# One fused attention and expert kernel: the experts' first block put through its first layer inside the attention's last batch, and the k and q stacks loaded one after the other

## What is computed

```python
for t in range(S):
    ar, ai = (a_re_n[:, :, t, :, None], a_im_n[:, :, t, :, None])
    new_re = ar * S_re - ai * S_im
    new_im = ar * S_im + ai * S_re
    kv = np.einsum('bhd,bhe->bhde', k[:, :, t], v[:, :, t])
    S_re, S_im = (new_re + kv, new_im)
    y[:, :, t] = np.einsum('bhd,bhde->bhe', q[:, :, t], S_re)
```

```python
logits = x @ w_gate + modality_bias[modality_id]
e_idx = np.argmax(logits, axis=1)
for e in range(E):
    mask = e_idx == e
    h = np.maximum(x[mask] @ w1[e], 0.0)
    out[mask] = gate_w[mask, None] * (h @ w2[e])
```

## Time and profile before

| what | value |
|---|---|
| median of three executions | 1009.62 us (1009.51 to 1011.83) |
| the profiled execution | 1016.24 us |
| its span, first to last instruction | 1014.5 us |
| PE busy | 826.1 us (81%) |
| DVE, ACT, POOL busy | 501.3, 345.9, 128.8 us |
| mean granted TensorE clock | 0.939 of full |

### The profile page before, as it was taken

The page is one execution under the profiler, slowest core; times in us unless marked ns, Lnnn a source line. Parts: engine busy times, 40 slices in busy tenths (PEclk is TensorE's granted clock), DMA queues, the critical chain, the costliest instruction groups (busy, mean ns, idle before and its releaser), DMA issues.

```text
span 1014.5 us, 11936 instructions
## 1 busy us (share of the span) xinstructions
PE 826.1 (81%) x4633; PEld 679.2 (67%) x4633; DVE 501.3 (49%) x920; ACT 345.9 (34%) x676; POOL 128.8 (13%) x126
## 2 busy tenths in 40 slices
PE   0059500399899997969999999989999999999996
PEld 0034200168788786838888888877898989898986
DVE  2599999959696853565345444544111111111110
ACT  6921101153535332425244524533222222222220
POOL 0201100000000302220000000000323232323232
PEclk9999855599897998989999999999999999999998
DMA  9934300475646456225244134214100000000000
GB/s 381 372 121 156 109 0 0 96 194 157 172 125 171 114 128 213 87 83 162 86 156 154 35 123 156 68 60 143 46 32 1 32 1 32 1 32 1 32 0 32
DMA packets 48054, 102.99 MB, mean 102 GB/s; under 512 B 12145, under 2 KB 30450, under 8 KB 45682
## 3 DMA queue, kind: packets, MB, share of 16 engines
q1 hardware_dynamic: 41810, 81.97, 26.3%
q0 software_dynamic: 5632, 18.94, 5.2%
q10 hardware_dynamic: 544, 1.20, 0.5%
HBM read 64.12 MB, written 18.95 MB: 82 GB/s over the span
## 4 chain that ended last, share of the span: by engine, by line
PE 69%; DVE 18%; ACT 5%; issue 3%; DMA 2%; another core or an unknown queue 1%; ACTq 1%; POOL 1%; SPq 0%; POOLq 0%; DVEq 0%
PE moe_bank L1573 18%; PE moe_bank L1574 18%; PE moe_bank L1575 18%; PE bank L989 4%; PE bank L1017 3%; DVE rows L783 3%; DVE rows L784 2%; PE bank L1034 2%; DVE gates L786 2%; PE bank L947 2%; PE bank L1038 1%; DVE gates L787 1%; DVE gates L773 1%; PE bank L997 1%; DMA gates<-a_im 1%
## 5 line engine op out<-in xcount | busy, mean ns | idle before, releaser
L1565 DVE TENSOR_TENSOR u_sb<-x_in,moe_bank 128x512 f32<-128x512 f32 x48 | 33.0, 688 | 229.9 <-PE moe_bank L1575 229.9
L1573 PE MATMUL moe_bank<-xT_hi,w_hi 128*128 128x512 f32 x312 | 124.1, 398 | 1.3 <-DVE xT_lo L1499 1.3
L1575 PE MATMUL moe_bank<-xT_hi,w_lo 128*128 128x512 f32 x312 | 123.8, 397 | 0.0
L1574 PE MATMUL moe_bank<-xT_lo,w_hi 128*128 128x512 f32 x312 | 123.5, 396 | 0.0
L1400 POOL TENSOR_TENSOR hid_lo<-u_sb,hid_hi 128x512 fp32r<-128x512 f32 x48 | 62.2, 1296 | 404.0 <-ACT hid_hi L1461 404.0
L960 PE MATMUL bank<-early_w_out,early_w3T 128*128 128x384 f32 x128 | 44.9, 507 | 64.7 <-DMA early_w_out<-w_out 61.3
L960 PEld LDWEIGHTS bank<-early_w_out,early_w3T 128*128 128x128 f32 x128 | 24.7, 197 | 84.4 <-issue 62.8
L952 PE MATMUL bank<-consts 128*128 128x512 f32 x36 | 18.4, 667 | 76.8 <-DVE gates L849 76.8
L1476 ACT COPY x_in<-moe_bank 128x512 f32<-128x512 f32 x48 | 28.3, 589 | 150.3 <-PE moe_bank L1575 150.3
L1439 ACT ACTIVATE hid_hi<-moe_bank 128x512 fp32r<-128x512 f32 x56 | 33.5, 597 | 129.2 <-PE moe_bank L1575 129.2
L1573 PE MATMUL moe_bank<-hid_hi,w_hi 128*128 128x512 f32 x168 | 67.5, 402 | 3.3 <-issue 3.3
(11 more groups left out here) (170 smaller groups left out, 1711.1 us busy)
## 6 DMA issues: line engine op xcount, KB each, us to landing
stage<-w SPq DMA_DIRECT2D x14, 1536.0 KB, 7.0
ks<-mags SPq DMA_DIRECT2D x48, 144.0 KB, 3.2
x_sorted<-early_zero POOLq DMA_DIRECT2D x8, 772.0 KB, 20.9
qs<-gates SPq DMA_DIRECT2D x42, 146.2 KB, 4.7
x_in<-x_sorted SPq DMA_DIRECT2D x28, 193.0 KB, 3.2
gates<-a_re SPq DMA_DIRECT2D x4, 1170.0 KB, 12.2
gates<-a_im SPq DMA_DIRECT2D x4, 1170.0 KB, 14.6
spare<-k SPq DMA_DIRECT2D x4, 1152.0 KB, 5.8
```

Source lines behind the costliest of these rows:

```text
L1565: nc.vector.tensor_tensor(u_sb[:, f % 2], a_sb[:, f % 2], bank_b[f % 2][:, :], ALU.mult).then_inc(u_ready, 1)
L1573: nc.tensor.matmul(out, l_hi, r_hi, start=first, stop=False)
L1574: nc.tensor.matmul(out, l_hi, r_lo, start=False, stop=False)
L1575: return nc.tensor.matmul(out, l_lo, r_hi, start=False, stop=last)
```

## The change

- `first` marks experts that have at least 512 tokens after two batches and prefers them; the lowest of them becomes block 0, whose 512 rows then all lie among the first two batches' rows. If there is none, a flag makes the table run block 0's entry again as a step (14 entries, `again_step`).
- SyncE, in the last batch: the store and reload of the smallest value now stand between the last unit's k and v loads and its q stack. Then come w1 of the first expert (when the last q stack has landed), block 0's four x loads, w2 and the order's store. For batches 1 to 3 each q stack waits until that unit's k stack has landed.
- `first` moves from slot 3 to slot 1 of the last batch, gate and place of the second batch from 1 to 2, the choice of the third batch from 2 to 3, the flag from 7 to 5, the choice of the last batch's four tiles from 12 to 13, their gate behind the loop.
- ScalarE scales block 0's x in slots 6 and 7, and splits w1 in slots 8 to 10 and half of w2 in 10 and 11. VectorE's low parts stand beside, some of them between scores and turned state.
- TensorE transposes x in the last unit's sixth chunk ahead of the sums, into banks of the attention. After the last unit it runs block 0's first layer, while VectorE routes the last tiles; the table is written in five pieces with a low part of the hidden layer after each. The eight matmuls on constants are gone. The engines wait for the table behind the branch of the fallback, and TensorE loads two registers there before its first step.
- Second batch's scatters are counted apart (`sorted_early`), and GpSimd waits for x's loads ahead of the third batch's. In every later block the transposes stand after the second output group instead of the first. Buffers are laid out anew.

The diff, cut to its core (unchanged helpers that only became functions are left out):

```diff
@@ first()
-        red(first_of, is_first, ALU.max)
-        ts(is_first, L.rcst("descend"), first_of, ALU.is_equal)
+        ts(whole, counts, float(BLOCK), ALU.is_ge, float(E), ALU.mult)
...
         tt(is_first, is_first, L.rcst("descend"), ALU.mult)
+        tt(whole, whole, is_first, ALU.add)
+        red(first_of, whole, ALU.max)
+        ts(L.scal[:, 12:13], first_of, float(E) + 0.5, ALU.is_lt)
+        ts(is_first, whole, first_of, ALU.is_equal)
...
@@ attention, sync
                     stack_k(b, m)
                     load_v(b, m)
+                    if b == B - 1 and m == NU - 1:
+                        sp.wait_ge(least_ready, 1)
+                        sp.dma_start(io["least"], L.least[:, :]).then_inc(least_out, DMA)
+                        sp.wait_ge(least_out, DMA)
+                        sp.dma_start(L.least_row[:, :], io["least"].rearrange("p o -> o p"),
+                                     allow_slow_non_contiguous=True).then_inc(least_in, DMA)
+                    sp.wait_ge(ks_in[m], (b + 1) * (DMA * n_ks))
                     if m == 0:
                         sp.wait_ge(qt_ready, stage_of(b) + 1)
                     stack_q(sp, b, m)
...
+            sp.wait_ge(qs_in[NU - 1], B * (DMA * n_qs))
+            sp.dma_start(L.stage1[:, :, :], io["w1"][bass.ds(e, 1)].rearrange("a (k p) f -> p (a k) f", p=P)).then_inc(W.w1_in, DMA)
+            sp.wait_ge(R.sorted_early, L.groups[1][1] * DMA)
+            load_x(sp, L, io, W, row)
+            sp.dma_start(L.stage2[:, :, :], io["w2"][bass.ds(e, 1)].rearrange("a (k p) f -> p (a k) f", p=P)).then_inc(W.w2_in, DMA)
+            keep_order(sp, L, io, W, 0, slice(0, BLOCK))
@@ attention, scalar, prepare
+                    elif slot in (6, 7):
+                        for q in (2 * (slot - 6), 2 * (slot - 6) + 1):
+                            scale_x(nc, act, L, W, 0, q)
+                    elif slot in EARLY_W1_HI:
                         if slot == 8:
                             act.wait_ge(W.w1_in, DMA)
...
@@ attention, scalar, behind the units
             route_exp(nc, act, L, R, B)
+            for f in range(KF):
+                hidden_high(nc, act, L, W, bank_scores[f % 2][:, :], 0, f)
+                if f >= 4:
+                    split_w2_hi(nc, L, f, W.w2_hi_ready)
@@ attention, vector, behind the units
+            V.gate(B - 1)
+            V.read_rank(B - 1, rank)
+            V.place(B - 1)
             V.choose(B)
-            V.read_rank(B - 1, late_rank)
-            V.place(B - 1)
+            first_low(0)
             V.gate(B)
-            V.read_rank(B, rank, True)
+            first_low(1)
+            V.read_rank(B, late_rank, True)
             V.place(B)
-            V.tables()
+            V.table_blocks()
+            first_low(2)
+            V.table_steps()
+            first_low(3)
...
+            V.table_rows()
+            first_low(6)
+            V.table_store()
+            first_low(7)
+            for f in range(4, KF):
+                split_w2_lo(nc, dve, L, f, W.w2_hi_ready, f + 1, W.w2_lo_ready)
@@ attention, tensor
+                        if n == B * NU - 1 and c == NCH - 1:
+                            pe.wait_ge(scores_ready, n * NCH + c)
+                            pe.wait_ge(krows_ready, n * (NCH - 1) + c)
+                            turn_x(nc, pe, L, W, first_xT, 0)
...
+            route_ranks(nc, pe, L, R, B - 1, rank)
             turn_y(B * NU * NCH - 1)
-            route_ranks(nc, pe, L, R, B - 1, late_rank)
-            route_ranks(nc, pe, L, R, B, rank)
+            for f in range(KF):
+                hidden(nc, pe, L, W, bank_scores, 0, f)
+                if f == 1:
+                    route_ranks(nc, pe, L, R, B, late_rank)
@@ experts, tensor
             def step(j):
                 output(j - 1, 0)
-                turn_x(j)
                 output(j - 1, 1)
+                turn_x(nc, pe, L, W, bank_xT, j)
                 output(j - 1, 2)
...
-            for _ in range(8):
-                nc.tensor.matmul(bank_hid[0][:, :], ident, L.const[:, 0:BLOCK], start=True, stop=True)
-            turn_x(0)
-            hidden(0)
-            each_step(pe, 1, step)
-            last8 = total(pe, L.NM8, KF, 1)
-            last3 = total(pe, L.NM3, KD, 1)
+            pe.wait_ge(R.table_ready, 1)
+            last8, last3 = total(pe, L.NM8, KF, 1), total(pe, L.NM3, KD, 1)
+            each_step(pe, step)
```

More of the change, by code:

```diff
@@ L333, in first, with again, over_j, table_blocks @@
         tt(L.prec[:, 0], key.unsqueeze(1).broadcast_to(ee), key.unsqueeze(2).broadcast_to(ee), ALU.is_lt)
-    def tables():
+    def again():
+        done(nc.vector.memset(L.scal[:, 12:13], 1.0))
+    again_step = L.scal[:, 12:13]
+    je = [P, NS, E]
+    step, steps = L.j13[:, 7], L.scal[:, 2:3]
+    row, off, expert, run, stj, sbj, block = (L.j13[:, i] for i in range(7))
+    most = L.j13[:, 8]
+    m0, m1 = L.m3[:, 0], L.m3[:, 1]
+    def over_j(a):
+        return a.unsqueeze(1).broadcast_to(je)
+    def table_blocks():
         edges = [P, E, L.rcst("edge").shape[1]]
@@ L346, in tables, with table_steps @@
         tt(se, sb_, nb, ALU.add)
-        steps = L.scal[:, 2:3]
+    def table_steps():
         red(steps, nb, ALU.add)
-        je = [P, NS, E]
-        over_j = lambda a: a.unsqueeze(1).broadcast_to(je)
-        step = L.rcst("step")
-        row, off, expert, run, stj, sbj, block, most = (L.j13[:, i] for i in range(8))
-        m0, m1 = L.m3[:, 0], L.m3[:, 1]
+        ts(step, L.rcst("step"), again_step, ALU.subtract)
         tt(m0, step.unsqueeze(2).broadcast_to(je), over_j(sb_), ALU.is_ge)
@@ L357, in tables, with table_pick, table_rows @@
         ts(se, counts, -float(BLOCK), ALU.add, 0.0, ALU.max)
-        for out, values in ((expert, L.rcst("expert")), (stj, st), (sbj, sb_), (most, se)):
+        ts(run, step, steps, ALU.is_lt)
+    def table_pick(which):
+        for out, values in ((expert, L.rcst("expert")), (stj, st), (sbj, sb_), (most, se))[which]:
             tt(m1, m0, over_j(values), ALU.mult)
             red(out, m1, ALU.add)
+    def table_rows():
         tt(block, step, sbj, ALU.subtract)
@@ new lines, in turn_x, with hidden_high @@
+def turn_x(nc, pe, L, W, banks, j):
+    for q in range(BLOCK // CH):
+        pe.wait_ge(W.x_scaled, j * (BLOCK // CH) + q + 1)
+        for k, bank in enumerate(banks):
+            mm = nc.tensor.transpose(bank[:, q * CH:(q + 1) * CH], L.x_in[:, q, k * P:(k + 1) * P], L.const[:, 0:P])
+            if q == BLOCK // CH - 1:
+                mm.then_inc(W.xT_psum, 1)
+def hidden_high(nc, act, L, W, bank, j, f):
+    act.wait_ge(W.hid_psum, j * L.hid_hi.shape[1] + (f + 1))
+    nc.scalar.activation(L.hid_hi[:, f], bank, ACT.Relu).then_inc(W.hid_hi_ready, 1)
@@ new lines, in hidden_low, with split_matmul @@
+def hidden_low(nc, dve, L, W, bank, j, f):
+    dve.wait_ge(W.hid_hi_ready, j * L.hid_hi.shape[1] + (f + 1))
+    nc.vector.scalar_tensor_tensor(out=L.hid_lo[:, f], in0=bank, scalar=0.0, in1=L.hid_hi[:, f].bitcast(F32), op0=ALU.max,
+                                   op1=ALU.subtract).then_inc(W.hid_lo_ready, 1)
+def split_matmul(nc, out, l_hi, l_lo, r_hi, r_lo, first, last):
+    nc.tensor.matmul(out, l_hi, r_hi, start=first, stop=False)
+    nc.tensor.matmul(out, l_hi, r_lo, start=False, stop=False)
+    return nc.tensor.matmul(out, l_lo, r_hi, start=False, stop=last)
@@ new lines, in hidden @@
+def hidden(nc, pe, L, W, banks, j, f):
+    KD, KF = L.xT_hi.shape[1], L.hid_hi.shape[1]
+    cols = slice(f * P, (f + 1) * P)
+    if f >= 2:
+        pe.wait_ge(W.hid_lo_ready, j * KF + f - 1)
+    pe.wait_ge(W.w1_lo_ready, j * KF + f + 1)
+    for k in range(KD):
+        if f == 0:
+            pe.wait_ge(W.xT_lo_ready, j * KD + k + 1)
+        mm = split_matmul(nc, banks[f % 2][:, :], L.w1_hi[:, k, cols], L.w1_lo[:, k, cols], L.xT_hi[:, k], L.xT_lo[:, k],
+                          k == 0, k == KD - 1)
+    mm.then_inc(W.hid_psum, 1)
@@ new lines, in load_x, with keep_order @@
+def load_x(sp, L, io, W, row):
+    for q in range(BLOCK // CH):
+        sp.dma_start(L.x_in[:, q], io["x_sorted"][bass.ds(row + q * CH, CH), :]).then_inc(W.x_loaded[q], DMA)
+def keep_order(sp, L, io, W, j, rows):
+    DM = L.shapes["w1"][1]
+    for q in range(BLOCK // CH):
+        sp.wait_ge(W.x_loaded[q], j * DMA + DMA)
+    sp.dma_start(io["order"][rows, 0:1].rearrange("(q p) o -> p q o", p=P), L.x_in[:, :, DM:DM + 1],
+                 allow_slow_non_contiguous=True).then_inc(W.order_kept, DMA)
@@ L1372, in step @@
                              ).then_inc(w2_in, DMA)
-            row = entry(L.ROW0, E * N - BLOCK)
-            sp.wait_ge(R.sorted_stored, NT * DMA)
-            load_x(row)
-            for q in range(BT):
-                sp.wait_ge(x_loaded[q], DMA)
-            sp.dma_start(io["order"][0:BLOCK, 0:1].rearrange("(q p) o -> p q o", p=P),
-                         x_in[:, :, DM:DM + 1], allow_slow_non_contiguous=True).then_inc(order_kept, DMA)
```

(4 more changed lines are left out.)

334 lines of the change are left out of this document (166 added, 168 removed).

## The result

The kernel after takes 998.3 us (median of four executions, 994.4 to 1000.7), the kernel before 1009.6 (1008.6 to 1011.8): a ratio of 0.988, with a 95% interval of 0.985 to 0.992, so 11.3 us less. The forecast was 996.1 in a range of 990.0 to 1008.5. The profiled execution after took 1000.67 (span 998.9), against 1016.24 (span 1014.5): 15.6 less, where the sum said 13.5.

The account below looks back on a forecast made before the run. TensorE has hardly a gap from 510 us, so only the wait between attention and experts could shrink: -12.4 there, -1.1 on attention's side, -13.5 from 1016.24 gives 1002.7; from the median 1009.62, 996.1, range 990 to 1008.5.

Parts of the forecast that it names:

- steps 1, 2: Around attention's end: twelve transposes end attention 1.0 later, at 433.4; VectorE sets the table's pace, ready at 454.0.
- steps 3, 4: Block 0's hidden layer, paced by VectorE, ends at 453.0; then 4.4 for the fallback branch and 1.4 for register loads.
- cheap branch: Rival, chance 0.13: TensorE's fallback branch is cheap, as on ScalarE, and no clock is lost: 4.8 better, 991.4.
- step 5: Block 0's output layer, behind the branch gap: 3 us at half clock, 1.4 lost, without the warming matmuls.
- Block 1's inputs: Block 1's x and weights: ready 22.0 behind the table, at 476.0, ahead of 478.3, so cost 0; margin 2.3.
- Behind that the sequence is the same before and after: From block 1's hidden layer to the end: nothing changes, so time saved is the amount that layer's start moves.
- Step 4: Between block 0's hidden and output layer: the fallback branch comes into the open, 4.4, plus two register loads, 1.4.
- The new chain on SP: Last batch's loads: x lands between 403.7 and 408.9, ScalarE waits for it, last unit's sums 1.5 earlier; net -1.1.
- covers it: Last batch: the profiled stall (ScalarE 7.15 us, TensorE 5.55) lies beside SP's new chain, which therefore hides in it.
- The stall's rival: Chance 0.27: the stall is the profiled execution's own; last unit's sums then stood at 401.7 and x delays them: 1006.6.
- The slower rival: Chance 0.08: ScalarE's wait for x at its worst, last unit's sums at 413.8, 12.1 behind 401.7: 1012.7.
- turning point of 9: Last unit: the change turns slower where its sums come more than 9 us behind 401.7.

Follow-up runs that it names:

- e12: The kernel of e11 with six matmuls on constants between TensorE's branch and its wait for the table: 999.4 us against 999.0.
- e5: The kernel after without the fallback recurrence and its branch in TensorE's program, only a wait for the flag: 1000.5 us (one execution).
- e3: The kernel after without SP's wait for the k stack ahead of each q stack: 996.1 us, 0.986 of before.
- e11: The kernel after with ScalarE's scalings of x moved to the last unit's third and fourth chunk: 999.0 us against 997.7 for the kernel after.
- e10: The kernel before with SP's w2 load behind the landing of w1: 1015.1 us against 1014.2, 1.000.
- e1: The kernel before, unchanged, profiled once more: 1013.4 us (one execution), beside a kernel before of 1010.0.
- e2: The kernel before with SP's wait for the k stack ahead of each q stack added: 1012.0 us, 1.002 of before.
- e4: The kernel after with SP's wait for the least value's store, and its load, behind the last q stack: 995.9 us, 0.985 of before.
- e9: The kernel after, unchanged, measured again: 997.7 us against 1014.2 for the kernel before, 0.984.
- e7: The kernel after with the least value's wait behind the last q stack, scalings late, and x, w2 each loaded after the previous landing: 996.5 us, 0.980.
- e8: The kernel after with block 1's w1 load issued ahead of its x loads: 995.8 us (one execution).

## Why the prediction was right, and where it wasn't

**The size was right, and partly by luck.** Two errors cancel. The tail and what follows gained 21.2 where the sum had 13.4, attention's side lost 2.2 where it had gained 0.1, and 3.4 were the execution's own start.

*Transposes and table (steps 1, 2).* The table came 20.1 behind attention's end for 20.6, and VectorE paced it. These held.

*Branch (steps 3, 4): mis-placed.* I had the hidden layer end 1.0 ahead of the table and then charged 4.4 us for the branch and 1.4 for the loads. The hidden layer did end 0.7 ahead, the loads took 1.4, and the branch's duration held, 4.2 to 4.7 from the flag's load on. What failed is where it begins: TensorE's queue runs ahead of its matmuls, so it reads the flag 2.7 us before the last one ends. Behind the table 0.8 of the branch is left, and the output layer came 2.3 us behind the table for 4.8; in e12 1.85 of the branch was in the open, and e5 took 0.5 to 1.0 off. The Trainium skill, "Runtime: NRT & Kernel Launch", section "Instruction fetch mechanics", has a taken branch to a page outside the window wait for a fetch. The trace agrees that the jump is long, 3.3 to 3.8 us in thirteen traces; whether a fetch fills it no run shows. That the queue may pay it ahead of the engine is what I left out. The rival "cheap branch" had 4.8 less; here it is 2.5 less and no clock lost, 3.9, so its price came near, for another reason.

*Clock (step 5).* 1.4 was charged. Nothing was paid in the profiled execution, e3 and e11, and 1.3 to 2.7 in the six others without the warming matmuls.

*Block 1's inputs.* 0 was charged, 1.34 paid in that execution and none in the others. The low parts of x were there 21.7 behind the table (458.02 to 479.76) for the 22.0 of the sum. TensorE came sooner than the sum had it, since branch and clock took 3.9 less, and with that the margin of 2.3 was gone.

*Behind block 1: the step that failed most.* "Behind that the sequence is the same before and after" was wrong. The two register loads for the last totals (L1623 and L1624 before) stood behind the loop, in the open. The change has them ahead of it, at 458.9, in the wait behind the table. Step 4 charged 1.4 for them there and gave nothing back where they went away. The 4.6 are these parts:

- Ahead of the first matmul behind the exit, 1.8 (3.33 and 1.52). Some 1.2 of it are the loads. 0.6 is the exit branch, 3.85 for 3.27, which was 3.43 to 3.85 in the four traces of the kernel before and its variants, and 3.25 to 3.71 in the ten of after and its. The whole gap was 2.97 to 3.33 in the four and 1.43 to 1.92 in the ten.
- The clock, 1.7. It was 0.79 from 686 to 694 in the profile of before, and likewise in e10; in e1 and e2 it stayed at 1.00, and the last stretch was 2.0 shorter. It was lost behind the longer gaps (3.33 and 3.24) and not behind the shorter ones (2.99 and 2.97), and in one of the ten of after and its (e4, 1.90). How much of it the shorter gap saves in most executions isn't known; against e1 and e2 the last stretch gained 2.7.
- Five steps, 0.8: 34.85 us each before, 34.71 after (34.62 the first). Why a step is shorter wasn't tried.
- 0.3 is spread over the last part.

That the loads are what moved is read from the queue. No run moves them alone.

*The new chain on SP: the wait was right, what follows it wasn't.* ScalarE waits for x ahead of the last unit and TensorE for its k rows, as said. The store took 9.7 for 7.7. But from its issue to x's scaling it was 26.5 us (384.11 to 410.58), inside the 23.3 to 28.5 of the sum, which reckons from 380.4. Counted from the first cut the last unit's sums start 0.9 earlier than before (32.2 for 33.1), where the sum had 1.5. What it put at nothing is the clock behind that wait, which two of its rivals priced at 2.5 and 3.0. The clock is 0.50 from 412 to 421, and it was 1.00 there before. From its first sums the last unit took 3.0 longer, where transposes and scalings had 1.4.

Whether the wait costs depends on the stall. With it, e9, x is in time and attention's side is level with before, as the forecast's "covers it" has it. Without it, the kernel after loses 7.3 in column 2.

*The stall's rival* was right that the stall is not in each execution: the profiled one stood 6.6 above the median, and that median is like the one beside e1. Its 401.7 for the last unit's sums was right too, 25.0 behind the first cut for e1's 24.9. Its price was not. It let the kernel before run through from there, but e1 then waits 3.2 for w1, at a clock of 0.57 behind it. Against that attention's side costs the change 7.0 (57.9 less 51.0; 3.9 by e3), where the rival had 10.4 with the transposes, and the tail and the exit pay more than I had: 998.3 instead of 1006.6.

*The slower rival* named the right mechanism, x at its worst. The sums stood 10.5 behind 401.7, but 3.4 of that is the execution's later start; counted from the first cut it is some 7, short of its turning point of 9.

**What stays open:** what the stall is, what the order of ScalarE is worth without it, and how much of attention's 2.2 is this one execution's clock.

## What to carry to other kernels

Cut both traces at a handful of points that exist in both, and take a second trace of the unchanged kernel before a stall is priced: here one event of 5 to 7 us made the reference 4.8 longer, and it covered another wait. Compare positions only when they are counted from such a point: a start 3.4 later looked like a longer chain. A branch is paid in an engine's queue, which may be ahead of its matmuls; what is in the open is the rest behind the last long instruction. Read a diff for loads and waits that move across a loop's end: I charged two register loads where they came to stand and gave nothing back where they had stood. And a middle over two transfers is neither one's landing.

## What the runs showed of the hardware

- **A stall of all engines at once.** In nine of fourteen traces ScalarE (4.4 to 7.2 us), VectorE (3.6 to 5.1) and TensorE (4.0 to 5.6) stand together in the last unit but one. TensorE waits for ScalarE's state; for the other two the profile names no engine and no transfer. In e9 ScalarE stands 5.08 [above] and VectorE 3.60:

```profile
390.64 0.69 DVE L1070 TENSOR_TENSOR scores<-bank,consts 128x512 f32<-128x512 f32 x1 [3.60 <-remote]
```

  GpSimd is issuing six indirect scatters just then:

```profile
383.17 0.96 POOL L442 DMA_INDIRECT x_sorted<-gates,pos_i  x1 [0.30 <-issue]
...
388.24 0.96 POOL L442 DMA_INDIRECT x_sorted<-gates,pos_i  x1 [0.31 <-issue]
```

  The kernel after issues the same six from 387.10 without a stall, so they alone don't make it. It was in none of the traces of e1 to e4, measured together, and in all of e5 to e12. Shorter ones (1.5 to 4.0 us on ScalarE) stand beside or just behind the next scatters in before, e5, e7, e8, e11 and e12, all of which have the first one too. The cause wasn't found.
- **A small store behind full queues.** 0.5 KB was seen landed 9.7, 8.9, 8.6 and 9.0 us behind its issue (after, e3, e11, e9), in the kernel after with a DMA share of 0.65 to 0.87. In e1 and e2 it was 7.0.
- **The same branch, long on one engine only.** The jump over the fallback took 3.3 to 3.8 us in TensorE's queue (thirteen traces) and the loop's exit 3.3 to 3.9 (fourteen), where the same loop branch, not taken, took 0.08. On ScalarE and VectorE these branches took 0.04 to 0.07.
- **The clock after a gap is not one number.** Behind idle times of 2.5 to 3.5 us at the same place TensorE's granted clock stayed at 1.00 in three traces (after, e3, e11) and fell to 0.50 for a time in six (e4 to e9), at a cost of 1.3 to 2.7 us. The idle times of the two groups overlap (3.00 to 3.40 and 2.50 to 3.45).
